# Attention, expert choice and experts in one kernel: DVE writes the first query tile's value means, and the first batch's expert choice moves to the last step of attention

## What is computed

```python
k_sum = k.reshape(B, H, nb, block, D).max(axis=3)      # block = 32, nb = 24
v_sum = v.reshape(B, H, nb, block, D).mean(axis=3)
scores_l = where(|pos - pos'| < 16, scale * q @ k.T, -1e9)
scores_s = scale * q @ k_sum.T + log(block)
a = softmax(concat(scores_l, scores_s))
attn = a @ concat(v, v_sum)
x = attn rows, 1536 x 512
logits = x @ w_gate                                    # 1536 x 8
# all (token, expert) pairs in order of falling logit: a token takes the first
# expert that still has room (192 places each)
y[tokens of e] = relu(x[tokens of e] @ w1[e]) @ w2[e]
h = y @ w_in;  s = h * softmax(h);  out = ((s - mean) / std * g_ln) @ w_out
```

## Times and profile before

| | us |
|---|---|
| median of three runs | 493.04 (492.8 to 493.86) |
| the profiled execution | 491.6 |
| its span, first to last instruction | 489.8 |
| PE busy in it | 472.2 (96%) |
| DVE busy | 341.7 (70%) |
| ACT busy | 170.7 (35%) |
| POOL busy | 136.9 (28%) |
| mean granted TensorE clock | 0.995 |

### The profile page before, as it was taken

How to read it: one execution, slowest core, us unless ns; L and a number is a source line. 1 busy time by engine, 2 the same in 40 slices (tenths; PEclk the granted TensorE clock), 3 DMA queues, 4 the chain that set the end, 5 groups by cost and what they waited for, 6 DMA issues and landing times.

```text
span 489.8 us, 8510 instructions
## 1 busy us (share of the span) xinstructions
PE 472.2 (96%) x3022; PEld 413.8 (84%) x3022; DVE 341.7 (70%) x1108; ACT 170.7 (35%) x354; POOL 136.9 (28%) x213
## 2 busy tenths in 40 slices
PE   8999999999999999999999999999999999999992
PEld 5888788788899899779989988998997899899871
DVE  5777777789888998999689779968966600400451
ACT  4677778633133211432222133322311331220340
POOL 5677777510310400141131112113112141010110
PEclk9999999999999999999999999999999999999998
DMA  8978872110450630091450045045105437000001
GB/s 262 323 247 267 266 251 77 33 33 0 177 201 0 217 162 1 7 371 43 171 195 33 15 181 202 23 169 187 42 12 197 189 127 272 0 23 0 1 21 43
DMA packets 30040, 61.75 MB, mean 126 GB/s; under 512 B 6576, under 2 KB 19760, under 8 KB 25904
## 3 DMA queue, kind: packets, MB, share of 16 engines
q0 software_dynamic: 6592, 39.85, 22.3%
q1 hardware_dynamic: 22544, 20.53, 13.3%
q10 hardware_dynamic: 864, 0.84, 0.6%
HBM read 54.93 MB, written 6.29 MB: 125 GB/s over the span
## 4 chain that ended last, share of the span: by engine, by line
PE 90%; DVE 5%; issue 2%; ACT 1%; DMA 1%; POOL 0%; DVEq 0%; POOLq 0%
PE psum L1157 17%; PE psum L1174 14%; PE psum L1264 6%; PE psum L1239 5%; PE psum L945 5%; PE psum L1246 5%; PE psum L1240 4%; PE psum L1208 4%; PE psum L954 4%; PE psum L1209 4%; PE psum L1218 4%; PE psum L980 4%; PE psum L977 2%; PE psum L1106 2%; PE psum L1186 2%
## 5 line engine op out<-in xcount | busy, mean ns | idle before, releaser
L1174 PE MATMUL psum<-xs,w_sb 128*128 128x192 f32 x512 | 87.0, 328 | 0.0
L1157 PE MATMUL psum<-shared,w_sb 128*128 128x192 f32 x512 | 84.6, 326 | 0.0
L1157 PEld LDWEIGHTS psum<-shared,w_sb 128*128 128x128 f32 x512 | 83.5, 190 | 1.1 <-issue 0.6
L1174 PEld LDWEIGHTS psum<-xs,w_sb 128*128 128x128 f32 x512 | 83.0, 190 | 0.0
L1546 DVE TENSOR_SCALAR_CACHE_REDUCE key_wide<-keys,thr 128x1536 bf16<-128x1536 f32 x35 | 63.3, 1808 | 0.6
L694 POOL DMA_INDIRECT w_sb<-w,widx x32 | 31.4, 982 | 95.5 <-DVE widx L1639 65.5
L718 POOL TENSOR_TENSOR gain<-spread,cst 128x1 f32<-128x1 f32 x12 | 6.8, 563 | 163.4 <-DVE spread L1701 163.4
L1668 DVE TENSOR_TENSOR yT_lo<-psum,yT_hi 128x384 fp32r<-128x384 f32 x16 | 8.8, 554 | 52.0 <-ACT yT_hi L824 51.8
L1239 PE MATMUL psum<-wout_hi,turned_hi 128*128 128x512 f32 x96 | 38.6, 402 | 0.7 <-ACT turned_hi L824 0.7
L777 ACT ACTIVATE keys<-keys,nmax 128x184 f32<-128x184 f32 x96 | 37.3, 439 | 4.7 <-DVE nmax L1378 4.7
L1208 PE MATMUL psum<-win_hi,yT_hi 128*128 128x512 f32 x96 | 38.6, 402 | 0.0
(11 more groups left out here) (186 smaller groups left out, 846.6 us busy)
## 6 DMA issues: line engine op xcount, KB each, us to landing
shared<-vT SPq DMA_DIRECT2D x8, 384.0 KB, 6.0
shared<-v_main SPq DMA_DIRECT2D x8, 384.0 KB, 3.6
x_rows<-xs SPq DMA_DIRECT2D x8, 384.0 KB, 4.6
shared<-kT SPq DMA_DIRECT2D x7, 384.0 KB, 5.9
shared<-qT SPq DMA_DIRECT2D x7, 384.0 KB, 5.4
w_sb<-w_in SPq DMA_DIRECT2D x4, 512.0 KB, 4.9
w_sb<-w_out SPq DMA_DIRECT2D x8, 256.0 KB, 4.2
w_sb<-v_tail SPq DMA_DIRECT2D x16, 48.0 KB, 3.4
```

Of the source, the lines that this page charges most:

```text
L1157: mm = pe.matmul(turn[u % 2][:, i * CAP:(i + 1) * CAP], w1_sb[:, par, first:first + P], xT[:, c, :], start=(c == 0), stop=(c == KC - 1))
L1174: mm = pe.matmul(turn[u % 2][:, (d % 2) * CAP:(d % 2 + 1) * CAP], w2_sb[:, par, first:first + P], hT[:, c, :], start=(c == 0), stop=(c == ...
```

## The change

DVE gets a function `first_value_mean`, called in step 2 ahead of `value_mean(0)`: it scales the turned sums straight from PSUM into tile 0 of `vt_sb`, for both heads, and raises a new semaphore. `values(0)` waits for that one. POOL's `value_summaries(0)` fills tiles 1 to 5 only, and `values(1)` waits for it.

`best_logit` is split: the maximum stays in step 43, and the comparison becomes `with_best_logit`. For batch 0 this, `preferred`, `first_keys` and the spreading of tiles 0 to 3 run at the end of step 47 (`UNITS - 1`). The spreading of tiles 4 and 5 and `experts_above(0)` run in step 50 (`UNITS + 2`), behind the last `normalise`. Steps 44 and 45 have no such work any more. The order for batch 1 is unchanged.

```diff
@@ value_summaries (POOL)
+                first = 0 if g else 1
                 for h, row in enumerate((TAIL, D)):
                     cols = slice(2 + h * D, 2 + h * D + D)
-                    pool.tensor_copy(vt_sb[row:row + NBLK, g % 2, :, cols],
-                                     over_query_tiles(vmean[row:row + NBLK, :], NBLK, D)).then_inc(vtail_ready, 1)
+                    pool.tensor_copy(vt_sb[row:row + NBLK, g % 2, first:, cols],
+                                     over_query_tiles(vmean[row:row + NBLK, :], NBLK, D, QT - first)).then_inc(vtail_ready, 1)
@@ values (PE)
                 if t == 0:
                     pe.wait_ge(in_v[b], 48 * (g // 2 + 1))
-                    pe.wait_ge(vtail_ready, 2 * g + 2)
-                    if g == 0:
+                    if g:
+                        pe.wait_ge(vtail_ready, 2 * g + 2)
+                    else:
+                        pe.wait_ge(vfirst_ready, 2)
                         pe.wait_ge(v_ones, 3)
                         pe.wait_ge(v_set, 2)
...
                 if u == 1:
                     pe.wait_ge(vmean_ready, 2)
+                    pe.wait_ge(vtail_ready, 2)
@@ DVE
+            def first_value_mean():
+
+                dve.wait_ge(vsumT_ready, 1)
+                dve.wait_ge(v_zeroed, 2)
+                for h, row in enumerate((TAIL, D)):
+                    dve.tensor_scalar(vt_sb[row:row + NBLK, 0, 0, 2 + h * D:2 + h * D + D], vsumT[:, h * D:h * D + D],
+                                      1.0 / BLOCK, None, ALU.mult).then_inc(vfirst_ready, 1)
...
                     if u == 2:
+                        first_value_mean()
                         value_mean(0, it)
...
             def best_logit(b):
                 link(dve.tensor_reduce(best[:, batch(b)], logit[:, batch(b), :], AX.X, ALU.max))
+
+            def with_best_logit(b):
                 link(dve.tensor_tensor(pick[:, batch(b), :], logit[:, batch(b), :], over_experts(best[:, batch(b)], QT),
                                        ALU.is_equal))
...
                 if u == EARLY_TURN:
                     best_logit(0)
-                if u == EARLY_TURN + 1:
+                if u == UNITS - 1:
+                    with_best_logit(0)
                     preferred(0)
-                if u == EARLY_TURN + 2:
                     first_keys(0)
-                if u == EARLY_TURN + 4:
                     spread_tiles(0, 4).then_inc(keys_ready, 1)
+                if u == UNITS + 2:
                     spread_tiles(4, QT)
                     experts_above(0)
```

More of the change, by code:

```diff
@@ L348, in build @@
         vmean_ready = sem("vmean_ready")
+        vfirst_ready = sem("vfirst_ready")
         vtail_ready = sem("vtail_ready")
@@ L536, in _, with over_query_tiles @@
             pool.memset(vt_sb[D:P, :, :, VCOLS - 1:VCOLS], 1.0).then_inc(v_ones, 1)
-            def over_query_tiles(ap, rows, width):
-                return ap.rearrange("p (o c) -> p o c", o=1).broadcast_to([rows, QT, width])
+            def over_query_tiles(ap, rows, width, tiles=QT):
+                return ap.rearrange("p (o c) -> p o c", o=1).broadcast_to([rows, tiles, width])
             def copy_first(h, count, first, second=None):
@@ L1449, in first_choice @@
                 best_logit(b)
+                with_best_logit(b)
                 preferred(b)
```

## The result

| | before | after |
|---|---|---|
| median, first measurement (3, then 4 runs of before; 4 of after) | 493.04, then 492.98 | 489.56 (489.35 to 489.82) |
| ratio | | 0.9927 (0.991 to 0.9945) |
| median, second measurement (35 runs of before, 12 of after) | 491.76 | 490.06 |
| ratio | | 0.9960 (0.9945 to 0.9976) |
| profiled execution | 491.6 | 489.82 |

But the forecast was a gain, 1.72 us, set against the median 493.04, and the kernel before has no single time: its executions form two groups, around 491.5 and around 493.0 us, which differ by one short fall of TensorE's clock. By their times (their clocks are not on record) the three runs shown ahead of the prediction, and the fourth that came with the result, were of the upper group, while the profiled execution, with a clock of 0.995, was of the lower.

The account below looks back on a forecast made before the run. The prediction took the kernel to be a queue of PE matmuls, gaining only where PE stops: 0.57 + 1.33 - 0.03 - 0.15 = 1.72 us off the 493.04 median, giving 491.3 us, range 490.4 to 492.7.

Parts of the forecast that it names:

- The stop at 11.13: PE's 0.85 us idle before `values(0)`, read as waiting for POOL's two value copies; it was to vanish.
- The other candidate: The first value DMAs, instead of POOL's copies, as what releases PE from its stop before `values(0)`.
- The cover of `values(1)`: POOL's copies were to end between 12.15 and 12.33, before `values(1)` at 12.6: 0.3 us of cover.
- Part one's gain: First value means made by DVE: 0.57 us gained up to `scores(6)`, with DVE's mask 5 last; bounds 0 and 1.09.
- rival (a): Part one gives little, PE paying DVE's 0.46 or POOL's later windows in full: total 1.15 to 1.3; 17 in 100.
- rival (b): Part one gives all its 1.09 us, mask 5 not being last: total 2.2, time 490.8; 8 in 100.
- Steps 44 to 46: PE's stops there go when the choice, mostly waiting for POOL, leaves: `scores(44)` to `scores(47)` 1.33 us shorter.
- Rival (d): PE is held in steps 44 to 46 by something else: total 0.3 to 0.6, time 492.6; 7 in 100.
- Step 47: The choice's five operations take 1.21 us here, nearly covered by DVE's idle; `invert(45)` slightly late, 0.03 charged.
- Behind step 50: Added DVE work is covered with 0.45 to spare; POOL's ranking now meets DVE's second choice, costing 0.15 us.
- (c): The wait for POOL returns behind step 50 at its full 0.8 us: total 1.1, time 492.0; 10 in 100.
- (e): Slower: no cover behind step 47, DVE the bound until the second choice: 0.7 us slower, 493.7; 5 in 100.

Follow-up runs that it names:

- after_again: The changed kernel measured once more, nothing altered: median 490.06 us, ratio to before 0.9960.
- pool_late: The changed kernel with two small fills added on POOL between the first value copies and the key windows: 491.30 us, one execution.
- act_means: The changed kernel with ScalarE, not DVE, making all four first value means: median 489.51 us, ratio to before 0.9945.
- split_later: The kernel before with POOL's last three splits of `w_out` moved behind its second ranking of experts: median 494.32 us, ratio to before 1.0046.
- after_delayed: The changed kernel with seven filling matmuls, not three, before the second batch's keys: median 491.43 us, ratio to before 0.9991.
- choice_alone: The kernel before with only the first batch's choice moved to step 47 and behind, value means as before: median 490.33 us, ratio to before 0.9972.

## Why the prediction was right and wrong

**Where it was wrong: the last line of the sum.** "The same 1.72 off the median gives 491.3." The 1.72 was worked out from an execution without a fall and taken off a median of executions that, by their times, all had one. The prediction saw that the profiled execution lay 1.4 us under the median of the runs and passed over it: it put at nothing, without a reason, that the executions after the change could be of the other group. Taken off 491.47, the median of before without a fall, the 1.72 gives 489.75; after_again without a fall has 490.05 and the first four runs 489.56, and why these two differ by half a microsecond is open. All four runs after the change had clocks of 0.992 to 0.995, so no fall. The first measurement's 3.48 us are so 1.57 for a fall, and 1.9 for the change, of which the second measurement has 1.4 (without falls). The kernels with part two had a fall in 15 of 100 executions and the others in 45. So four runs without one come in half of such measurements, and three of three with one, which misled the forecast, in about 9 of 100: that part was bad luck. The range of 490.4 to 492.7 had no place for a second group.

**Also put at nothing: the time outside the span.** The prediction took the same 1.72 off the span and off the time. Part one adds 0.25 us outside the span, so that its 0.38 is worth little more than 0.1 in the time. That the profiled execution took 489.82 where 489.9 was forecast is luck: the stretch gave 0.08 less than forecast, the time outside the span took 0.25, and 0.4 more went behind the second keys, which the prediction held unchanged.

**The stop at 11.13: right.** With tile 0 no longer from POOL's copies, it vanished, and `values(0)` starts at 10.95 with the same DMAs. The other candidate was close: in pool_late, where `scores(3)` is 0.65 us earlier, the profile names the DMA of `v_tail` for an idle of 0.17 us there. The cover of `values(1)` held.

**Part one's gain: mechanism half right, 0.57 against 0.38.** The three gaps of DVE closed as reckoned: mask 5 moved by 0.59, even more than 0.47. But "DVE ends last" failed. POOL was put "much as DVE does" at 15.7. Its windows do start 0.37 later (12.31 against 11.94), within the 0.3 to 0.45 forecast, and its last copy ends at 15.59; but PE starts 0.25 us behind that, where the 15.7 left at most 0.2. act_means and pool_late show it. So rival (a) had the right engine, POOL, and too high a price for it, and rival (b) falls: `scores(6)` is not free.

**Steps 44 to 46: right to the hundredth.** 1.33 us, and split_later shows that it was all waiting for POOL. Rival (d) falls.

**Step 47: right.** Five operations in 1.20 us (1.21); `invert(45)` has no gap before it. From `scores(47)` to the last addition it is 7.18 us after and 7.17 before, so 0.01 where 0.03 was charged.

**Behind step 50: right in kind, smaller in size.** POOL's ranking does meet the second choice, and one tensor_tensor is longer by 0.05, not 0.15. The added operations hid, with 0.51 to spare (0.45). Rivals (c) and (e) fall. The sum by the traces: 0.38 + 1.33 - 0.01 - 0.05 = 1.65, against 1.72.

**Behind the second keys** the prediction had a sign of its own for being wrong, a change of more than 0.3 us, and it is met: 387.33 us before and 386.95 after. Executions of the kernel before without a fall have 387.3 to 387.5 there. The profiles with the first means made early and no fall have 386.8 to 387.1, but for after_delayed with 387.5, and choice_alone has 387.4. With one profile for each kernel this shows no cause, and it stays open.

## What to carry to other kernels

Before taking a gain off a median, ask why the profiled execution differs from the timed ones: a tuned kernel can have one place where TensorE's clock falls in some executions, worth as much as the change, and three runs can all be of one kind. Look for such a place at an idle of PE, here behind two-column matmuls, and fill it if filling costs nothing. Compare time less span as well: here two DVE instructions came with 0.25 us that no timeline shows. When a short DVE operation is several times as long as its twin on other data, look for a POOL operation that ends just before it: moving either away wins the whole wait, but what is moved has to land where the other engine is quiet.

## What the runs showed of the hardware that was not expected

- The device time was 1.75 to 1.88 us longer than the span in the kernels whose DVE does not run `first_value_mean`, and 2.0 to 2.25 us in those where it does.
- PE's waiting matmul started 0.25 us after the end of POOL's last copy at `scores(6)` (15.59 to 15.84), and 0.11 us after it at `values(0)` of the kernel before; why these differ is open. The profile may name another engine as the releaser meanwhile.
- In split_later DVE's tensor_scalar has the earlier start in the records (109.12, POOL's 109.15) and still takes three times its usual time, ending 0.35 us behind POOL. The order of the recorded starts does not tell who waits.
